# ScalarE's affine step takes its scale from a register instead of from SBUF

## What is computed

```python
kv_flat = kv_pool.reshape(B, -1, C) @ w_sr        # 768 keys; k = v = kv_flat
a = np.exp(s - s.max(-1, keepdims=True)); a /= a.sum(-1, keepdims=True) + 1e-09
x = (a @ v)                                       # s = q @ k.T / sqrt(128)
x = np.maximum(x @ w_in, 0.0) ** 2 @ w_out        # first layer
h = x @ w_in2                                     # second layer
P = a[0] + a[1] * h + a[2] * h2 + a[3] * h3       # h2 = h*h, h3 = h2*h
Q = 1.0 + np.abs(b[0]) * np.abs(h) + np.abs(b[1]) * h2
out = (P / (Q + 1e-6)) @ w_out2
```

## Time and profile before

| | before |
|---|---|
| device time, 3 runs | 1526.04 us median (1525.57 to 1528.15) |
| the profiled execution's own time | 1526.38 us |
| its span in the trace | 1524.3 us |
| granted TensorE clock, mean | 0.999 of full speed |
| PE busy | 1492.0 us, 98% |
| DVE busy | 1458.7 us, 96% |
| ACT busy | 1389.8 us, 91% |
| POOL busy | 1193.4 us, 78% |

### The profile page before, as it was taken

One profiled execution on the slowest core, in us unless ns is written; L12 is line 12 of the kernel. 1 busy time (PEld: TensorE's weight loads), 2 busy tenths in 40 slices (PEclk: granted clock), 3 DMA queues, 4 the chain that ended last, 5 costly groups with the idle time before them and its releaser, 6 DMA issues.

```text
span 1524.3 us, 20377 instructions
## 1 busy us (share of the span) xinstructions
PE 1492.0 (98%) x5553; PEld 985.5 (65%) x5553; DVE 1458.7 (96%) x2572; ACT 1389.8 (91%) x2626; POOL 1193.4 (78%) x1179
## 2 busy tenths in 40 slices
PE   5999999999999999999999999999999999999987
PEld 4999999765665666656666566666666665666655
DVE  7888888889999999999999999999999999999998
ACT  3777777699999999999999999999999999999997
POOL 4544445358888888888888889888988888898887
PEclk9999999999999999999999999999999999999999
DMA  6201001000000000000000000000000000000000
GB/s 223 83 21 28 21 28 42 1 1 1 8 8 8 8 0 8 8 8 1 8 7 8 1 8 8 8 0 8 8 8 0 8 8 8 8 1 8 8 8 7
DMA packets 11517, 24.19 MB, mean 16 GB/s; under 512 B 1440, under 2 KB 2336, under 8 KB 11168
## 3 DMA queue, kind: packets, MB, share of 16 engines
q1 hardware_dynamic: 11424, 23.14, 4.6%
HBM read 16.85 MB, written 6.29 MB: 15 GB/s over the span
## 4 chain that ended last, share of the span: by engine, by line
PE 82%; DVE 10%; ACT 3%; issue 2%; POOL 2%; DMA 1%; SPq 0%; POOLq 0%; ACTq 0%; DVEq 0%
PE psum L933 18%; PE psum L902 18%; PE psum L765 10%; PE psum L766 10%; PE psum L767 10%; PE psum L854 6%; PE psum L817 6%; PE psum L839 4%; DVE tb L695 2%; DVE tb L718 2%; DVE tb L701 2%; DVE psum L706 2%; DVE g1h L681 1%; DMA X<-kvT 1%; POOL tb L393 1%
## 5 line engine op out<-in xcount | busy, mean ns | idle before, releaser
L395 POOL TENSOR_TENSOR wb<-wb,ub 128x512 f32<-128x512 f32 x384 | 496.7, 1293 | 31.3
L387 POOL TENSOR_SCALAR wb<-ub,babs 128x512 f32<-128x512 f32 x384 | 297.2, 774 | 104.2 <-ACT ub L518 104.2
L902 PE MATMUL psum<-tb,wout 128*128 128x512 f32 x736 | 376.8, 594 | 0.9 <-DVE tb L750 0.9
L933 PE MATMUL psum<-g,wout 128*128 128x512 f32 x736 | 375.9, 592 | 0.5 <-ACT x2f L503 0.5
L519 ACT ACTIVATE tb<-psum,ca 128x512 f32<-128x512 f32 x384 | 310.6, 809 | 0.0
L765 PE MATMUL psum<-x2h,win2h 128*128 128x512 f32 x384 | 290.3, 756 | 2.5 <-POOL x2l L380 2.4
L701 DVE SCALAR_TENSOR_TENSOR tb<-tb,ca,psum 128x512 f32<-128x512 f32 x365 | 269.3, 738 | 0.0
L695 DVE SCALAR_TENSOR_TENSOR tb<-tb,ca,psum 128x512 f32<-128x512 f32 x364 | 267.8, 736 | 1.5 <-ACT psum L552 0.8
L536 ACT ACTIVATE lnb<-wb 128x512 f32<-128x512 f32 x384 | 255.0, 664 | 4.6 <-POOL wb L395 4.0
L518 ACT ACTIVATE ub<-psum 128x512 f32<-128x512 f32 x384 | 239.1, 623 | 21.2 <-PE psum L767 14.0
L933 PEld LDWEIGHTS psum<-g,wout 128*128 128x128 f32 x736 | 139.7, 190 | 175.0 <-issue 168.2
(11 more groups left out here) (107 smaller groups left out, 2375.0 us busy)
## 6 DMA issues: line engine op xcount, KB each, us to landing
qraw<-qT SPq DMA_DIRECT2D x23, 256.0 KB, 2.7
outT<-osb SPq DMA_DIRECT2D x23, 256.0 KB, 2.0
X<-kvT SPq DMA_DIRECT2D x15, 384.0 KB, 7.6
wraw<-w_in SPq DMA_DIRECT2D x2, 1024.0 KB, 8.3
X<-kvT SPq DMA_DIRECT2D x2, 192.0 KB, 10.4
outT<-osb SPq DMA_DIRECT2D x2, 128.0 KB, 1.8
qraw<-qT SPq DMA_DIRECT2D x1, 192.0 KB, 10.1
wsr<-w_sr SPq DMA_DIRECT2D x1, 64.0 KB, 1.9
```

The costliest lines, as they stand in the source:

```text
L387: nc.gpsimd.tensor_scalar(w, u, babs[:, 1:2], babs[:, 0:1], ALU.mult, ALU.add).then_inc(v_rdy, 1)
L395: nc.gpsimd.tensor_tensor(w, w, u, ALU.mult).then_inc(w_rdy, 1)
L902: mm(ACC2, wout2[:, f, :], tb[:, t % T_RING, :], start=(f == 0), stop=(f == NF - 1))\
L933: mm(ACC1, wout1[:, f, :], g1[:, t % G_RING, :], start=(f == 0), stop=(f == NF - 1))\
```

## The change

Once, ahead of stage B's loop, ACT loads a3 from SBUF into a register of its sequencer. T1 then names the register as its scale. Its bias stays the column in SBUF. All 384 T1 instructions change; nothing else does.

```diff
             act.wait_ge(pv_rdy, NCH)
             act.wait_ge(ql_rdy, NCH)
             act.wait_ge(coef_in, 32)
+            a3 = act.alloc_register("a3")
+            nc.scalar.reg_load(a3, ca[0:1, 3:4].bitcast(mybir.dt.int32))
...
                     nc.scalar.activation(tb[:, t % T_RING, :], h2(t), ACT.Identity,
                                          bias=ca[:, 2:3],
-                                         scale=ca[:, 3:4]).then_inc(t1_rdy, 1)
+                                         scale=a3).then_inc(t1_rdy, 1)
```

## The result

The changed kernel takes 1524.13 us, median of 22 runs (1521.46 to 1525.04), against 1526.01 us (1525.39 to 1528.15, 22 runs) of the kernel before. The ratio is 0.9984, with a 95% interval of 0.9978 to 0.999: 0.16% faster, 0.10% to 0.22%.

What follows compares the result with a forecast made beforehand. PE was taken as the bound, with a 0.1 us stall per chunk end waiting for x2l. Terms -2.0 - 0.3 - 0.65 - 0.1 + 0.2 = -2.85 us gave 1523.2 us, range 1521.4 to 1526.6.

Steps and rivals of the forecast that it cites:

- T1's length: ACT's T1 instruction: dropping one column operand gains 0.09 us a T1, the register costing the engine nothing.
- The steady part: Chunk ends: x2l starts about 0.13 us earlier, so PE's 0.1 us stall goes whole at 21 ends, 2.0 us gained.
- Rival A: Chunk ends: x2l doesn't come early enough, for instance since POOL keeps its time; PE's stall stays, 1525.2 us, chance 0.15.
- Rival D: Steady part: all PE steps take the shorter 3.113 us, and DVE is ahead by 0.8 us; 1521.6 us, chance 0.20.
- The last chunk's end: First layer's last chunk: DVE, ahead by its lost stalls, brings x2h earlier; 0.3 us gained, ends 0 and 1.1.
- The last blocks: T1 on the chain eight times; DVE's slack limits each period's shrinking to 0.08 us, 0.65 us gained.
- The ramp: Where the steady steps begin: T1 is on the chain once, 0.1 us gained, with the first chunk's end.
- The load: Register load ahead of stage B's first relu: costs between nothing and 1.75 us, taken as +0.2.
- Rivals B and C: T1: B, register doesn't shorten it, 1526.0 to 1526.3, chance 0.10; C, register makes it longer, 1531.3 at +0.1 us, chance 0.10.

Runs made afterwards that it cites:

- e1_again: The changed kernel run again with no edit, against the kernel before: 1522.02 us (5 runs) against 1527.14, ratio 0.9966.
- the ends: Register only in T1s around chunk ends (block mod 16 from 11 to 15), column elsewhere, against the kernel before: 1525.35 us against 1526.54, ratio 0.9989.
- the middle kernels: Register only in 110 T1s in the middle of chunks (block mod 16 from 2 to 6), against the kernel before: 1526.55 us against 1526.54, ratio 0.9999.

## Why the prediction was right

1523.2 us was forecast and 1524.13 measured, a gain of 2.8 us against 1.9. The mechanism was the one named; one term was of the wrong kind, and several were a little off. That the median came as near as 0.9 us is in part luck: none of the 22 runs lies within 0.7 us of 1523.2, the forecast stands between the two groups, and the median depends on how many runs fall in each. In the five runs of `e1_again` all fell in the lower one, 5.1 us under the kernel before on that chip.

*T1's length*: right. 0.10 start to start against 0.09, and the register is free, as the lower bound had it.

*The steady part, -2.0*: the step was right and is shown by the ends and the middle kernels. The stall went whole, as forecast: `x2l` 0.17 earlier against a stall of 0.1, where 0.13 was forecast. Rival A, that POOL keeps its time, fell with it. What failed is that the forecast took the rest of PE's time as fixed. It is 3.113 or 3.12 a step, and the kernel before had both, by turns. Rival D saw this but took it to be a gain only. The runs show either: with the stalls gone, PE keeps one cadence for the whole execution. At 3.113 the 21 chunks give 3.24 us, at 3.12 only 1049.33 - 1048.32 = 1.01. So the forecast of 2.0, with the mixture kept, lies between the two and is met by neither; the lower group comes near D's time (1522.0 against 1521.6), for D's first reason alone, since DVE ahead by 0.8 us didn't come; the median lies in the upper group.

*The last chunk's end, -0.3*: measured -0.13, and in the upper group 48.82 (1465.77 - 1416.95), -0.20. Too large by 0.1 to 0.2, and for a reason: DVE was to come ahead by its lost stalls, but PE came forward with it. Where the kernel before has exp waiting 0.52 us for DVE ahead of `x2h`, the changed kernel has 0.56 in the lower group and 0.41 in the upper:

```profile
1460.29 0.60 ACT L554 ACTIVATE psum<-lnb 128x512 f32<-128x512 f32 x1 [0.56 <-DVE tb L737]
```

```profile
1462.71 0.60 ACT L554 ACTIVATE psum<-lnb 128x512 f32<-128x512 f32 x1 [0.41 <-DVE tb L737]
```

*The last blocks, -0.65*: measured -0.77 with all T1s and -0.70 with these alone. DVE's slack did bound the period, at 5.62 where 5.64 was read.

*The ramp, -0.1*: measured -0.35 from attention's last copy to the first mark, of which 0.08 is the relu's start. Nearly all of the other 0.27 is three of PE's steps ahead of the first mark, each 0.08 or 0.09 shorter (2.52, 3.20 and 4.42 before, 2.44, 3.11 and 4.34 after), where the forecast counted one.

*The load, +0.2*: wrong in sign, by little. It took 0.46 us and was hidden beside the copy, and the relu behind it started 0.08 sooner. The Trainium skill, "Runtime: NRT & Kernel Launch", section "The ~15µs preamble/postamble breakdown", gives its 1.3 us for register loads from HBM; here one register is loaded, from SBUF, in 0.46 us. The Trainium skill, "DMA: Bandwidth & Descriptors", section "Latency and other measured facts", puts the floor of a tensor load at about 600 ns, above the 457 to 465 ns measured here. Rivals B and C fell with the register's price.

*Slips in the working*: D's time is 1521.6 by its own sum, and the range begins at 1521.4; ten times C's 0.5 us is 5.2 by its terms, not 5.3; and the earlier trace rows hold steps of 3.21 and 3.11 alone, so they don't show D's two cadences, which the chunks of 50.01 and 49.92 do. None of it moves the forecast.

*Sum by the measured terms*: lower group -0.35 - 3.24 - 0.13 - 0.77 = -4.5 with +0.19 ahead of stage B; upper group -0.35 - 1.01 - 0.20 and 57.41 - (1522.4 - 1465.77) = 0.78, together -2.3 with +0.44 ahead.

## What to carry to other kernels

A scale that is the same on all partitions belongs in a register or a constant if ScalarE is anywhere on a chain: here it was worth 0.09 to 0.10 us an instruction, at the price of one load beside other work. Shortening an instruction that runs 384 times paid only in two places: where the shortened run ended at a buffer handed to the full engine, and in the ramp and the last blocks, where the instruction stood on the chain itself. So look for these places and count them, not the instructions. Where an engine's own cadence shows two values in one trace, take neither as fixed, and look at the single runs, not at the median alone. And where the chain passes from one engine to another between two profiles, compare the steps of the two engines before calling the new one the bound.

## What was not expected of the hardware

The full PE, doing the same six fp32r and two fp32 products a step with no wait of its matmuls in the profile, runs at 3.113 or at 3.12 us a step, 49.81 or 49.92 a chunk, at a granted clock of 0.998 to 1.0 either way. In the kernel before, the cadence changed only from one chunk to the next; without stalls it was the same through 21 chunks in all nine profiles (five of 49.81: the changed kernel three times, the one with one constant and the one with the early load; four of 49.92: the two single runs of the changed kernel, the one with two constants and the one with the register around the chunk ends), and it moves a run's time by 2.2 us. That the stall at a chunk's end is what lets it change is argued from this, not shown. DVE is not what sets it: its own step is 3.1105 us, and in the slower cadence it waits. What picks the cadence, and why there are two, stays open.
